# Windowed attention scores as 64x64 tiles of TensorE, one PSUM bank for each head

## The reference

```python
scores = 1/8 * q @ k.T            # per batch and head, 576 x 576
# heads 0-3: 0 <= i - j < 32;  heads 4-7: 0 <= i - j < 128 and (i - j) % 4 == 0
scores = where(mask, scores, -1e9)
p = exp(scores - max(scores)); x = (p / (sum(p) + 1e-9)) @ v       # -> [4, 576, 512]

xk = mu_k * x + (1 - mu_k) * x_prev;  xr = mu_r * x + (1 - mu_r) * x_prev
x = sigmoid(xr @ w_r) * (relu(xk @ w_k) ** 2 @ w_v)                # 512 -> 1024 -> 512

u = x + (x.T @ U @ V).T
out = u + relu(u @ w_ch1) @ w_ch2                                   # 512 -> 2048 -> 512
```

## Time and profile before

| | |
|---|---|
| median of three runs | 834.91 us |
| the profiled execution's own time | 836.28 us |
| its span, first to last instruction | 834.5 us |
| PE busy | 794.1 us (95%) |
| DVE busy | 323.6 us (39%) |
| ACT busy | 332.2 us (40%) |
| POOL busy | 152.1 us (18%) |
| mean granted clock of PE | 0.977 of full speed |

### The profile page before, as it was taken

How to read it: one execution, slowest core, us unless ns; L and a number is a source line. 1 busy time by engine, 2 the same in 40 slices (tenths; PEclk the granted TensorE clock), 3 DMA queues, 4 the chain that set the end, 5 groups by cost and what they waited for, 6 DMA issues and landing times.

```text
span 834.5 us, 13588 instructions
## 1 busy us (share of the span) xinstructions
PE 794.1 (95%) x5176; PEld 695.9 (83%) x5176; DVE 323.6 (39%) x660; ACT 332.2 (40%) x885; POOL 152.1 (18%) x169
## 2 busy tenths in 40 slices
PE   5579999989999999989999999999999999999998
PEld 4357888878888888877889899999989999999997
DVE  5556846464647463673541131121122113113111
ACT  5558676767676765552343211111111111111110
POOL 5694201030102012330056500000000000000000
PEclk8679999999999999998999999999999999999999
DMA  5544231023212200100023210000000000001001
GB/s 130 145 125 114 63 82 45 14 74 83 55 42 59 55 14 1 51 7 20 1 95 132 77 39 1 1 25 12 0 0 38 0 0 38 0 0 38 1 0 38
DMA packets 83349, 35.78 MB, mean 43 GB/s; under 512 B 71136, under 2 KB 77280, under 8 KB 83296
## 3 DMA queue, kind: packets, MB, share of 16 engines
q1 hardware_dynamic: 83296, 35.07, 15.3%
HBM read 30.33 MB, written 4.72 MB: 42 GB/s over the span
## 4 chain that ended last, share of the span: by engine, by line
PE 86%; DVE 4%; ACT 3%; POOL 2%; SPq 2%; issue 1%; DMA 1%; DVEq 0%; ACTq 0%; POOLq 0%
PE bank L1187 25%; PE bank L1189 25%; PE bank L1188 25%; PE bank L1226 3%; PE bank L1232 2%; PE bank L1241 2%; PE bank L1203 2%; SPq L449 1%; PE bank L1270 1%; DMA k_raw<-in_k_dram 1%; PE bank L1205 1%; DVE sq L1046 1%; PE bank L1329 1%; ACT probs L743 1%; POOL wr_l L622 1%
## 5 line engine op out<-in xcount | busy, mean ns | idle before, releaser
L925 ACT ACTIVATE h_h<-bank 128x384 fp32r<-128x384 f32 x96 | 47.2, 492 | 332.2 <-PE bank L1189 332.2
L1157 DVE SCALAR_TENSOR_TENSOR h_l<-bank,h_h 128x384 fp32r<-128x384 f32 x96 | 53.5, 557 | 308.9 <-ACT h_h L925 308.9
L1187 PE MATMUL bank<-ut_h,w_h 128*128 128x384 f32 x384 | 130.4, 340 | 0.0
L1189 PE MATMUL bank<-ut_h,w_l 128*128 128x384 f32 x384 | 129.3, 337 | 0.0
L1188 PE MATMUL bank<-ut_l,w_h 128*128 128x384 f32 x384 | 128.9, 336 | 0.0
L1189 PE MATMUL bank<-w_h,h_l 128*128 128x512 f32 x288 | 113.8, 395 | 0.0
L1188 PE MATMUL bank<-w_l,h_h 128*128 128x512 f32 x288 | 113.6, 394 | 0.0
L1187 PE MATMUL bank<-w_h,h_h 128*128 128x512 f32 x288 | 112.0, 389 | 0.0
L1187 PE MATMUL bank<-xs_h,wk_h 128*128 128x256 f32 x288 | 85.9, 298 | 0.7 <-DVE xs_l L1116 0.7
L1188 PE MATMUL bank<-xs_l,wk_h 128*128 128x256 f32 x288 | 81.6, 283 | 0.0
L1189 PE MATMUL bank<-xs_h,wk_l 128*128 128x256 f32 x288 | 81.4, 283 | 0.0
(11 more groups left out here) (126 smaller groups left out, 1341.3 us busy)
## 6 DMA issues: line engine op xcount, KB each, us to landing
stage<-in_moe_w_ch_dram SPq DMA_DIRECT2D x16, 512.0 KB, 3.3
out_dram<-result SPq DMA_DIRECT2D x18, 256.0 KB, 2.0
q_raw<-in_q_dram SPq DMA_DIRECT2D x64, 64.0 KB, 2.2
k_raw<-in_k_dram SPq DMA_DIRECT2D x64, 64.0 KB, 2.2
v_raw<-in_v_dram SPq DMA_DIRECT2D x32, 64.0 KB, 2.3
stage<-in_moe_w_k_dram SPq DMA_DIRECT2D x4, 512.0 KB, 4.2
stage<-in_moe_w_v_dram SPq DMA_DIRECT2D x4, 512.0 KB, 3.8
v_raw<-in_v_dram SPq DMA_DIRECT2D x16, 96.0 KB, 2.6
```

Of the source, the lines that this page charges most:

```text
L925: act.activation(h_h[:, m % KRING, :], h_bank[m % 2][:, 0:C2], ACT.Relu).then_inc(hh_done, 1)
L1157: dve.scalar_tensor_tensor(h_l[:, m % KRING, :], h_bank[m % 2][:, 0:C2], 0.0, h_h[:, m % KRING, :].bitcast(F32), op0=ALU.max, op1=ALU.subt ...
L1187: pe.matmul(dst, lhs[0], rhs[0], start=start, stop=False)
L1189: return pe.matmul(dst, lhs[1], rhs[0], start=False, stop=stop)
```

## The change

For every B step but those with the ends (24 of 32), the two heads become 64x64 tiles: head h takes rows 64h to 64h + 63 of `q_t` and of `k_t` alone and writes partitions 64h to 64h + 63 as before, and the heads write to two banks. So `banks_of` gives B two banks always, and the four banks go round faster: 208 uses instead of 184. Before its first matmul such a step waits until both banks are free. DVE's mask addition is done for each head on 64 partitions, so 24 additions are added. The eight B steps with the ends stay as they were (`with_ends`).

```diff
 def banks_of(step):
     if st == "B":
-        return 2 if DILATED[p] and k % 2 else 1
+        return 2
...
-                    wait_mm(dve, ("B", k, p, 0))
                     scores = probs[b][:, 0:nu * keys].rearrange("p (a b) -> p a b", b=keys)
-                    dve.tensor_tensor(scores, abank(("B", k, p, 0))[:, 0:nu * keys].rearrange("p (a b) -> p a b", b=keys),
-                                      m, ALU.add).then_inc(att_vector, 1)
+                    for h in range(1 if with_ends(k, p) else 2):
+                        rows = slice(0, P) if with_ends(k, p) else slice(DH * h, DH * h + DH)
+                        wait_mm(dve, ("B", k, p, h))
+                        dve.tensor_tensor(scores[rows], abank(("B", k, p, h))[rows, 0:nu * keys].rearrange("p (a b) -> p a b", b=keys),
+                                          m[rows], ALU.add).then_inc(att_vector, 1)
...
+            def scores_by_head(k, p):
+                n, dil, half = nth(k, p), DILATED[p], k % 2
+                for h in range(2):
+                    if GROUP["B", k, p, h] >= ABANKS:
+                        wait_drained(pe, GROUPS[GROUP["B", k, p, h] - ABANKS])
+                wait_drained(pe, ("A", k, p, 0))
+                wait_drained(pe, ("A", k, p, 1))
+                for i, (query, col, keys) in enumerate(units(k, p)):
+                    first_key = SUB * i if dil else FROM[half] + UQ * i
+                    for h in range(2):
+                        rows = slice(DH * h, DH * h + DH)
+                        ins = pe.matmul(abank(("B", k, p, h))[rows, col:col + keys], q_t[n % 2][rows, h, query:query + UQ],
+                                        k_t[p][rows, first_key:first_key + keys], start=True, stop=True)
+                        if i == len(units(k, p)) - 1:
+                            ins.then_inc(att_mm, 1)
+
             def attention(stage_, k, p):
                 n, dil, half = nth(k, p), DILATED[p], k % 2
+                if stage_ == "B" and not with_ends(k, p):
+                    scores_by_head(k, p)
+                    return
```

More of the change, by code:

```diff
@@ L101, in normalised_in, with with_ends @@
     return sorted([(k, p) for (st, k, p), n in SLOT_OF.items() if st == "C" and n == slot + 1])
+def with_ends(k, p):
+    return DILATED[p] and k % 2 == 1
 LAST_SLOT = max(SLOT_OF.values())
@@ L1211, in attention @@
                         for i, (query, col, keys) in enumerate(every):
-                            if (i == DILATION and dil) != (j == 1):
+                            if (i == DILATION) != (j == 1):
                                 continue
-                            if not dil:
-                                rhs = k_t[p][:, FROM[half] + UQ * i:FROM[half] + UQ * i + keys]
-                            elif keys == 2 * UK:
+                            if keys == 2 * UK:
                                 rhs = k_t[p][:, 0:S].rearrange("p (r j) -> p r j", r=DILATION)[:, :, SUB - UK // 2:SUB]
                             else:
-                                first_key = SUB * i + (JCUT - WINDOW if half else 0)
+                                first_key = SUB * i + JCUT - WINDOW
                                 rhs = k_t[p][:, first_key:first_key + keys]
```

## The result

The changed kernel takes 844.08 us (median of 5 runs, 842.93 to 844.81); the kernel before took 835.67 us beside it (834.12 to 838.01). The ratio is 1.0095 (95% interval 1.0072 to 1.0118), so it is slower by 0.7 to 1.2%. The forecast was 840.9 us and slower, with a range of 834 to 846. The direction and the places are right. The time is 3.2 us over the forecast: the added time was forecast 2.4 us too small (6.0, against 8.4 between the medians and 7.8 between the spans of the two profiled executions), and the kernel before took 0.8 us more beside the changed one than in the three runs on which the forecast stood (835.67 against 834.91).

A forecast was written before the change was run, and what follows sets the result against it. PE was taken as the bound (busy 794.1 of 834.5 us), DVE counting only where PE waits for it. Matmuls 0, shapes 1.05, DVE 2.8, banks 2.1 and start-up 0 gave +6.0 on 834.9: 840.9 us, range 834 to 846.

The forecast's parts named there:

- The matmuls: B steps on PE: no gain from narrower tiles, 0 us, bounds -7.2 to +14.3.
- half-length scores: Rival for B steps: 64x64 tiles on separate rows and columns run twice as fast; 833.7 us, chance 0.12.
- (c): Rival for B steps: tiles that differ in rows do not overlap; +14.3 us, 855.2 us, chance 0.06.
- the reading of rows 3 and 4: Profile rows of B and transposes: 0.46 against 0.82 ns a column, so the heads' records overlap in pairs in B.
- Changes of shape: PE between B and D: net 7 changes of tile shape at 0.15 us, +1.05 us, bounds 0 and 2.0.
- DVE before V7: Slot 9: second mask addition delays the squares V7 waits for; 0.5 or 0.6 us a chunk, none in chunk 2, +2.8 us.
- Banks in chunk 0: B(1, 2) waits 1.8 us for DVE's copy of k, plus +0.3 at D(1, 1): +2.1 us, bounds 0.5 and 3.
- D(1, 1): Chunk 0: waits 0.9 us for the first copy of C(1, 2), partly given back at D(1, 2): +0.3 us.
- the start-up: Additions of B(0, 0) to B(0, 3) before 32 us: 0, up to 1.5 us more if their cover were gone.
- Rival (b): DVE's second addition and the banks cost a third, shifting into DVE's idle time; 836.5 us as middle, chance 0.20.
- Marks named beforehand: Signs for the profile after: B step lengths, D's shifts, two 650 ns additions, V7's gap 0.6 us longer, waits before B(1, 2), D(1, 1).

The follow-up runs named there:

- Experiment 5: Kernel before with 64x64 tiles for the same 24 B steps, both heads in one bank and one mask addition: 835.33 us, ratio 0.9981.
- experiment 4: Kernel before with B's loop over heads outside the loop over blocks, so one head's matmuls follow the other's: 843.6 us, ratio 1.0092.
- experiment 1: Kernel before with DVE's mask addition split in two of 64 partitions each, from one bank: 838.48 us, ratio 1.0043.
- experiment 10: Changed kernel with unit 9's squares ahead of slot 9's attention and `xs_l` right behind B's mask and maximum on DVE: 837.68 us, ratio 1.0009.
- experiment 2: Changed kernel with B's matmuls over all 128 rows again, still two banks and two additions: 841.73 us, ratio 1.0075.
- experiment 3: Changed kernel with DVE's copy of k of A(1, 3) ahead of the squares in chunk 0, slot 2: 840.63 us, ratio 1.0063.
- experiment 8: Changed kernel with unit 9's squares ahead of slot 9's attention on DVE, chunks 0 to 5: 843.51 us, ratio 1.0079.
- experiment 6: Kernel before with unit 9's squares ahead of slot 9's attention on DVE, chunks 0 to 5: 836.1 us, ratio 0.9998.
- experiment 7: Kernel before with unit 9's squares ahead in slot 9 and one-bank 64x64 tiles only for plain pairs with even k: 835.41 us, ratio 0.9988.
- experiment 9: Kernel before with unit 9's squares ahead of slot 9's attention and `xs_l` right behind B's mask and maximum on DVE: 833.22 us, ratio 0.9958.
- experiment 11: Changed kernel with squares and `xs_l` ahead in slot 9, and k of A(1, 3) copied ahead of slot 2's squares in chunk 0: 834.72 us, ratio 0.9972.

## Why the prediction was right, and where its sizes were off

**The matmuls: right.** 0 was taken, and the B step of 20 records has its length (1.04 against 1.05 us). Experiment 5 excludes half-length scores and (c), +14.3 us for tiles on different rows; experiment 4 confirms by its direction the reading of rows 3 and 4, that two column tiles overlapped before. The prediction set aside a rule of the Trainium skill (TensorE: Matmul & The Clock Gate, Part 3, The mechanism) by which a weight load overlaps running matmuls only when its row group differs from theirs. The traces do not bear it out here: 20 loads of 0.15 us ran within 0.88 us on the same rows, and with separate rows for the heads the step is no shorter (1.04 us against 1.05). The Trainium skill (TensorEngine Tiling (Array Packing), Overview, Theoretical Speedup) gives up to 2x for a dimension of 64 or less. Here the rows brought nothing where the column tiles ran together already (1.04 against 1.05 us).

**Changes of shape: right in kind, somewhat too large in sum.** A change costs 0.15 us where it shows, as forecast. Outside slot 9 ten changes were added and three taken away; of these seven and one show in the comparison, a net of 6 and +0.9, less 0.2 in small steps: +0.7 where 1.05 was forecast. The added ones that don't show, B(4, 1), B(6, 1) and B(2, 0), stand before a wait for ACT.

**DVE before V7: a term that was mis-sized, 3.8 us for 2.8.** The mechanism and the places are right: all chunks pay but chunk 2, whose loss goes into the DMA wait (0.57 less 0.47). Two steps made it too small. I took 0.6 for the second addition from the overlap of unlike operations; from start to start it adds 0.69 (1.38 for two against 0.69 for one). And the copy of D behind the maximum starts 0.11 us later than it did, in experiment 1 as well (0.69 from the maximum to it against 0.57 before). This is so wherever the copy directly follows the maximum of a step with two additions, in the traces of all kernels that have such steps, and nowhere behind a single addition. Why, no run tells; in experiment 10, where `xs_l` stands behind the maximum, the step is 0.57.

**Banks in chunk 0: right place and releaser, 1.8 forecast and 3.3 measured.** This is the largest miss. The wait itself was sized rightly, 1.68 us of idle time. The rest, 1.6 us, is the clock at its 1.2 GHz level in B and behind it, a term that the prediction had not in its sum at all; "nothing gives it back" was right, but that the wait could cost more than its length was not considered. It does not each time (experiment 2). D(1, 1) is +0.34 for the +0.3 forecast.

**The errors partly cancel.** DVE +1.0 and the clock +1.6 were missing from the sum; the shapes were 0.35 too high, and the start-up (+0.56) and what is behind 325 us (-0.9) are no effect of the change. 844.08 us lies near the upper end of the 838 to 845 that the prediction gave from its bounds.

**Rival (b), the waits are covered,** is excluded by experiment 1, where the additions alone cost 3 us and more. Its idea that DVE has time enough is true in the sum and needs the right order: in experiment 10 the second addition no longer makes V7 or the next chunk wait, with two operations moved.

**Marks named beforehand.** B 0.88 us until the next step: 0.97, of which 0.09 is the change of shape. D behind B(3, 2) 0.1 us later: yes. Behind B(4, 2) earlier: yes, 0.56 us from the one to the other instead of 0.82. Two additions of 650 ns: yes (1.34 for the pair). V7 longer by 0.6 in chunks 1, 3 and 5: 0.64 to 0.65. B(1, 2) preceded by a wait over 1 us, for the k copy: yes, though the profile's row names ACT. D(1, 1): 0.75 us of idle time for `probs_t`.

## What to carry to other kernels

Before splitting a tile to gain speed, compare the time for a column in a step that uses one tile with that in the step to be changed (here 0.82 and 0.46 ns): if the second is about half, two tiles already run together, and here narrowing them brought nothing. Price an operation added on a lightly loaded engine by what is queued behind it where the busy engine already waits; and if two late results leave one queue at its end, moving one ahead only hands the wait to the other, so move both ahead of what nobody needs soon (the single move gave 0.9998, both 0.9958). Where banks go round faster, look for a use whose copy-out stands behind other work in its engine's queue, and reorder that.

## What the runs showed of the hardware

In these traces PE starts records out of program order where the next step's are for another tile. Where B and D both use 64*64, here B(2, 2) and D(2, 0) in chunk 0 of the changed kernel, D's first record starts before B's last three:

```profile
93.41 0.79 PE L1212 MATMUL bank<-k_t,q_t 64*64 64x96 f32 x13
93.96 0.27 PE L1268 MATMUL bank<-probs_t,v_raw 64*64 64x64 f32 x1
93.96 0.33 PE L1212 MATMUL bank<-k_t,q_t 64*64 64x96 f32 x3
94.07 0.68 PE L1268 MATMUL bank<-probs_t,v_raw 64*64 64x64 f32 x15
94.68 0.50 PE L1196 MATMUL bank<-wv_h,sq_h 128*128 128x512 f32 x1
```

B to the v block takes 94.68 - 93.41 = 1.27 us there, where a pair of steps of the same form took 171.90 - 170.47 = 1.43 before. Experiment 4 shows it within a step. It is why putting the heads one after the other made a B step of 20 records 0.55 us longer and not the 0.77 expected; the whole cost 8 us and not 21.

An addition of 480 columns costs 0.65 us on 64 partitions and 0.655 on 128: splitting by partitions doubles the cost. Two matmuls on different rows, each with its own partitions of one bank (experiment 5), ran beside each other as those on shared rows do.

An operation of DVE can take many times its length beside one of POOL. `sq_l` on 256 columns takes 0.42 us, but 2.49 us from 88.06 in the kernel before, beside POOL's `xs_l`, which runs from 87.81 to 90.26. In experiment 3 DVE starts first, at 88.41, and POOL at 88.45: there `sq_l` takes 0.43 us. In chunks 0, 2 and 4 this long operation stands ahead of the mask addition of slot 9, in the kernel before and in the changed one, and in chunk 0 of the changed kernel it makes V7 0.56 us later than in experiment 3. The prediction's account of slot 9 leaves it out.

The granted clock can fall behind a wait that is short. Four traces have the wait of 1.7 us before B(1, 2), all after a slow start. In three (the changed kernel, experiments 8 and 10) the clock fell for 3.4 to 6.8 us; there PE had come to the 2.4 GHz level 4.7 to 5.8 us before the wait began. In experiment 2 it did not fall. The clock records of that trace begin only at 49.8 us, but the spacing of the matmuls shows the slow start too (256 columns take 0.21 us until 49.6 and 0.12 behind it), 6.5 us before the wait. Near that place the clock fell in no trace without the wait. A slow start just before is not needed: between chunks 2 and 3, where PE had been at the 2.4 GHz level for 120 us and more, it fell for 3.4 us behind the wait for k from a DMA in experiments 6, 7 and 9 to 11 (waits of 2.2 to 3.0 us), but not in experiment 5 (2.5 us) nor in the other traces (1.0 to 1.6 us). In those five it takes back a part of what they gained. What decides it between executions stays open.
